# First batch's scores times values and state products on 32-column tiles of TensorE, in a kernel of decayed linear attention and two MLP blocks

## What is computed

```python
for t in range(S):
    state = alpha[:, :, t, :, None] * state + einsum('bhd,bhe->bhde', k[:, :, t], v[:, :, t])
    y[:, :, t] = einsum('bhd,bhde->bhe', q[:, :, t], state)
```

```python
u = x + (x^T @ U @ V)^T
x = u + relu(u @ w_ch1) @ w_ch2              # 384 -> 1536 -> 384
```

```python
h = relu(x @ w_in); u, v = halves of h       # 384 -> 2 x 512
gated = u * (w_spatial @ norm(v) + b_spatial)
out = gated @ w_out                          # 512 -> 384
```

## Time and profile before

| | before |
|---|---|
| median of 3 runs | 735.48 us (733.66 to 736.63) |
| profiled execution | 735.8 us, span 734.0 us |
| PE busy | 702.6 us (96%), 11336 matmul records |
| PEld busy | 663.7 us (90%) |
| DVE, ACT, POOL busy | 401.9 (55%), 338.6 (46%), 213.5 us (29%) |
| mean granted clock of PE | 0.993 of full |

### The profile page before, as it was taken

The page is one execution under the profiler, slowest core; times in us unless marked ns, Lnnn a source line. Parts: engine busy times, 40 slices in busy tenths (PEclk is TensorE's granted clock), DMA queues, the critical chain, the costliest instruction groups (busy, mean ns, idle before and its releaser), DMA issues.

```text
span 734.0 us, 25697 instructions
## 1 busy us (share of the span) xinstructions
PE 702.6 (96%) x11336; PEld 663.7 (90%) x11336; DVE 401.9 (55%) x668; ACT 338.6 (46%) x573; POOL 213.5 (29%) x141
## 2 busy tenths in 40 slices
PE   2689889999999999999999999999999999999998
PEld 2688789899899999999999999998998998999998
DVE  6889874554655455555453314224942851870671
ACT  5787446446536436446434421334532432532422
POOL 6500890320351220152120141452260051033022
PEclk9979999999999999999999999999999999999999
DMA  9414321211401131311010252002100101101001
GB/s 361 161 46 143 109 79 46 87 70 46 153 4 46 36 121 46 110 46 45 4 36 2 72 147 95 33 1 97 64 34 33 65 12 54 64 1 64 0 0 65
DMA packets 16525, 49.49 MB, mean 67 GB/s; under 512 B 1616, under 2 KB 9552, under 8 KB 15920
## 3 DMA queue, kind: packets, MB, share of 16 engines
q1 hardware_dynamic: 16432, 48.09, 18.7%
HBM read 38.65 MB, written 9.44 MB: 66 GB/s over the span
## 4 chain that ended last, share of the span: by engine, by line
PE 86%; DVE 1%; issue 1%; ACT 1%; DVEq 0%; ACTq 0%
PE HB L894 24%; PE ZB L982 7%; PE ZB L984 7%; PE ZB L983 7%; PE SB L894 6%; PE SB L1019 5%; PE SB L771 4%; PE ZB L894 4%; PE SB L1023 2%; PE ZB L1032 2%; PE ZB L1019 2%; PE SB L876 2%; PE SB L1032 2%; PE SB L885 1%; PE SB L831 1%; PE HB L1019 1%
## 5 line engine op out<-in xcount | busy, mean ns | idle before, releaser
L1543 DVE SCALAR_TENSOR_TENSOR hid_lo<-HB,hid_hi 128x384 fp32r<-128x384 f32 x92 | 51.2, 556 | 132.0 <-ACT hid_hi L1218 131.3
L1218 ACT ACTIVATE hid_hi<-HB 128x384 fp32r<-128x384 f32 x92 | 45.3, 492 | 146.3 <-PE HB L894 146.1
L894 PE MATMUL HB<-uh,w1h 128*128 128x384 f32 x276 | 98.8, 358 | 0.0
L982 PE MATMUL ZB<-hid_hi,w2h 128*128 128x384 f32 x288 | 98.6, 342 | 0.0
L984 PE MATMUL ZB<-hid_lo,w2h 128*128 128x384 f32 x288 | 96.7, 336 | 0.0
L983 PE MATMUL ZB<-hid_hi,w2l 128*128 128x384 f32 x288 | 96.3, 334 | 0.0
L894 PE MATMUL HB<-ul,w1h 128*128 128x384 f32 x276 | 92.9, 336 | 0.0
L894 PE MATMUL HB<-uh,w1l 128*128 128x384 f32 x276 | 92.6, 336 | 0.1
L1073 ACT COPY Qd<-Q 48x768 f32<-48x768 f32 x84 | 72.8, 867 | 21.8 <-POOL Q L662 8.4
L719 POOL TENSOR_TENSOR gl<-gf,gh 128x384 fp32r<-128x384 f32 x32 | 33.6, 1050 | 144.0 <-ACT gh L1258 143.8
L662 POOL TENSOR_TENSOR Q<-Q,bk 112x768 f32<-112x768 f32 x13 | 24.4, 1875 | 165.1 <-ACT Qd L1073 165.1
(11 more groups left out here) (268 smaller groups left out, 1529.0 us busy)
## 6 DMA issues: line engine op xcount, KB each, us to landing
Q<-in_q SPq DMA_DIRECT2D x8, 768.0 KB, 5.3
AL<-in_al SPq DMA_DIRECT2D x7, 768.0 KB, 4.4
K<-in_k SPq DMA_DIRECT2D x7, 768.0 KB, 4.3
Vt<-in_v SPq DMA_DIRECT2D x8, 576.0 KB, 3.6
mid<-x2s SPq DMA_DIRECT2D x8, 576.0 KB, 3.7
x<-mid SPq DMA_DIRECT2D x4, 1152.0 KB, 5.2
out<-o_sb SPq DMA_DIRECT2D x24, 192.0 KB, 1.8
x2s<-in_w SPq DMA_DIRECT2D x9, 384.0 KB, 4.2
```

Of the source, the lines that this page charges most:

```text
L894: last = nc.tensor.matmul(dst, weights(x, w), moving(y, m), start=(n == 0 and x == y == 0), stop=(n == total - 1 and y == 1))
L982: nc.tensor.matmul(bank, w2h[:, i, cols], hi, start=(i == 0), stop=False)
L1218: nc.scalar.activation(hid_hi[:, i % HID, :], up_bank(i)[:, 0:TILE], ACT.Relu).then_inc(h_hi, 1)
L1543: nc.vector.scalar_tensor_tensor(hid_lo[:, i % HID, :], up_bank(i)[:, 0:TILE], 0.0, hid_hi[:, i % HID, :].bitcast(F32), ALU.max, ALU.subtr ...
```

## The change

It takes the distinction of the first batch out of the two places. `first` no longer chooses the cut: L876 uses QUARTERS instead of HALVES, and L885 QUARTERS instead of WHOLE, in the first batch as in the others.

```diff
                         for hh in range(2):
                             o, e = o0 + HD * hh, p * PW + HD * hh
-                            for t in HALVES if first else QUARTERS:
+                            for t in QUARTERS:
                                 last = nc.tensor.matmul(w.YB[y][t, o:o + HD], w.A[:, u, hh, t], Vt[g][:, c, e:e + HD],
                                                         start=(m == p == hh == 0), stop=False, skip_group_check=True)
...
                         for m, p, c, u, o0 in output_blocks(y):
-                            for t in (WHOLE if first else QUARTERS) if c else []:
+                            for t in QUARTERS if c else []:
                                 last = nc.tensor.matmul(w.YB[y][t, o0:o0 + PW], Q[g][:, u * CH + t.start:u * CH + t.stop],
                                                         w.St[:, p, c - 1, :], start=False, stop=(m == p == 1),
                                                         skip_group_check=True)
```

## The result

The changed kernel is slower: 743.8 us median (742.4 to 745.4, four runs) against 734.6 us of the kernel before beside it (733.7 to 736.6, four runs). The ratio on record is 1.0118, with a 95% interval of 1.0093 to 1.0142 (the two medians by themselves give 1.0125). The forecast was 735.1, the range ended at 737.2.

What follows compares the result with a forecast made beforehand. The prediction took PE as the bound up to 63.54 us, then an ACT and DVE chain, and PE again from about 110 us. PE's 2.8 us shrank to 1.8, 0.8, then 0.4: median 735.1 us, range 733.2 to 737.2.

Steps and rivals of the forecast that it cites:

- the first two terms of the sum: First-batch L876 and L885 on PE: 1.70 us less over six steps and 1.08 us less over two groups.
- supply of instructions: Rival: PE stops for instructions inside L876 and L885; about 737.3 us with four or five stops, chance 0.08.
- That work is the same in both kernels: From about 110 us PE's own work sets the end, so an earlier gain carries through unchanged.
- the wait of Q's load for PE's group 0: Next batch's Q load: this wait passes earlier but is not the last one before the load's issue at 61.4 us.
- The chain behind PE: After L885, ACT's copies and DVE's L1533 hold L940; of PE's 2.8 us about 0.8 are left.
- the term: First L940: starts 0.8 us earlier, held by DVE's L1533.
- whole-gain rival: Rival: the chain behind L885 gives way and all 2.8 us count, 732.7 us; chance 0.08.
- The 0.4 us forecast at the end: Next batch's first scores wait for Q's copies, so 0.4 us is carried to about 110 us and the end.
- nothing arrives: Rival: Q lands later or a weight piece holds the next batch's chain, 71 to 110 us; 735.5 us, chance 0.16.
- The clock: Rival: PE's granted clock falls near 65 us, 2 to 4 us are lost, 739 us; chance 0.07.
- A fixed time per matmul: Rival: each record takes 31 ns whatever its width, L876 costs 5.9 us more, 741.4 us; chance 0.01.
- estimate by the floor of the Trainium skill: L876 and L885 at about 25 ns from start to start: 3.1 us more on PE; not used for the sum.

Runs made afterwards that it cites:

- e3: The changed kernel with L876's six first-batch steps as a loop, three turns over the two y = 0 steps (y = 1 and 2 left out); 737.83 us, ratio 1.0032.
- e6: The changed kernel with 36 small products of zeros (144 instructions) at the start of PE's program; 743.31 us, ratio 1.0113.
- e5: The kernel before with 28 small products of zeros (112 instructions) while PE waits for K; 740.46 us, ratio 1.0071.
- e8: The kernel before, its L876 steps still in halves but in the loop of e3; 735.69 us, ratio 1.0006.
- e7: The kernel of e3 with 36 small products of zeros (144 instructions) at the start; 735.77 us, ratio 1.0008.
- e1: The kernel before with only the first batch's L876 cut in quarters, L885 left whole; 743.75 us, ratio 1.0109.
- e9: The kernel of e1 with 32 small products of zeros (128 instructions) at the start; 742.84 us, ratio 1.0104.
- e10: The kernel before with only the first batch's L885 in quarters, plus 4 small products of zeros (16 instructions); 736.81 us, ratio 1.0025.
- e11: The changed kernel with K of batch 1 loaded after the first of three weight pieces instead of before it; 744.17 us, ratio 1.0136.

## Why the prediction was wrong, point by point

**L876 at 0.70 us a step, L885 at 1.78 (the first two terms of the sum).** This is the step that failed. The prices are right as rates of a burst: steps of 0.70 us stand in every kernel with the new form of L876, and e3 made six in 5.1 us, 0.85 each with the turns of its loop. They were taken from stretches that are followed by slow rows and used for one that is nearly four times as long. The count that mattered is instructions per us, weight loads among them. The ends of the stops are one block apart: 4.0, 4.7 and 3.7 us in the changed kernel, 3.7, 3.7, 4.7 and 3.7 in e6, so PE gets 256 instructions in 3.7 to 4.7 us, 54 to 69 per us (3.4 to 4.8 us over all runs). L876 in halves uses 64 in 0.98 us, 65 per us, just within it; in quarters 128 in 0.70 us, 183 per us. L885 in quarters uses 160 in 1.78 us, 90 per us, whole 40 in 2.3, 17 per us. The 1088 instructions of the stretch are 4.25 blocks, 16 to 20 us at this rate, which was read from the same stops; it took 68.92 - 51.86 = 17.1 us. The sum of -2.8 us on PE should have been +6.5.

**The rival "supply of instructions".** It was the right mechanism with the wrong size. It priced a stop at the 1.06 us of the earlier trace rows and allowed four or five, which gave 737.3 and a chance of 0.08. The stops were four, but of 0.8 to 2.6 us. The row of L819 gave the place where one block ends. Had the next ones been counted from it, 128 records apart, the kernel before would have shown how near the limit it was: its block inside L876 lasts 128 records at 29 ns, 3.7 us.

**"That work is the same in both kernels".** The instructions from 110 us on are the same, their place in the blocks isn't. 624 is 112 more than two blocks, and the tail is 2.3 us longer with that shift and not without it (e6); in e5 a shift of 112 made the kernel before 5 us slower. A busy PE after 110 us did not mean that nothing could come between. The prediction also had the wait of Q's load for PE's group 0 pass early; in the changed kernel the load goes out right behind that group, 5.1 us later than before, so nothing absorbed the delay.

**The chain behind PE.** In e3 PE goes from the start of L876 to L909 in 8.8 us, 1.8 less than before; DVE then holds L940 by 1.03 us, and the stage is 0.8 us shorter, which was the term. In e8 DVE holds it too, by 0.54 us. e7, where L940 waits for ACT, has a stage 0.5 us shorter than e8. So the whole-gain rival doesn't hold there; the changed kernel itself never reached this chain, since L1533 waited 6.0 us for ACT. The 0.4 us forecast at the end were not seen: e7 and e8 have medians within 0.1 us of each other, as the rival "nothing arrives" has it, though the scatter could hide 0.4 us.

**The Trainium skill on this.** It has the block (Runtime: NRT & Kernel Launch, Instruction fetch mechanics): 256 instructions, 16 KiB, fetched by the sequencer while the current block is executed. The spacing of the stops and the packets agree. It calls the cost of crossing a block mostly hidden; these runs disagree: where PE stopped at a crossing in this stretch, it was for 0.4 to 3.5 us.

**The other rivals.** The clock did fall, at 57 us, but behind the first stop; e6 has the loss without the fall. A fixed time per matmul was refuted in every run with the new form of L876: 64 records in 0.70 us. The prediction's estimate by the floor of the Trainium skill (TensorE: Matmul & The Clock Gate, Back-to-back issue gap) also applied it to L885, whose 96 moving columns lie outside the 1 to 64 that it names, so its 3.1 us are not what the page gives.

## What to carry to other kernels

Count instructions per microsecond, weight loads included, before cutting matmuls into smaller tiles. A burst of 144 records ran without a stop here; one of 544 ran at the rate at which instructions arrived, whatever the array could do, and its six steps of L876 took half the time in a loop. And when instructions are added anywhere in unrolled code, look for "issue" stops far behind them: compare with a copy whose total shift is a whole number of blocks before judging the change by its time.

## What was not expected of the hardware

- Between the ends of two stops PE got 256 instructions in 3.4 to 4.8 us (3.45 in e1, 4.8 in e9 and e10). Why the interval differs stays open; e11 doesn't settle whether data traffic is the reason.
- A shift of unchanged code by 112 instructions cost 5 us (0.7%, e5).
- The turns of a loop on PE started with stops of 0.17 to 0.19 us only (second and third turn in e3 and e7).
- 112 semaphore increments on PE kept it until 18.3 us, at most 0.16 us each if they began with the span (e4).
